# Half of an outer product from VectorE to ScalarE, and another order of the loads of the second layer's weights

## The reference

```python
X = np.fft.fft(x, axis=1); X = np.fft.fft(X, axis=2)      # x: (2, 3008, 256)
h = X.real.reshape(6016, 256) @ w_in                      # first layer, w_in: (256, 2048)
g = np.maximum(h, 0.0) ** 2
z = g @ w_out                                             # w_out: (2048, 256)
h = z @ w_in2                                             # second layer, same shapes
P = a[0] + a[1] * h + a[2] * h**2 + a[3] * h**3
Q = 1.0 + abs(b[0]) * abs(h) + abs(b[1]) * h**2
out = (P / (Q + 1e-06)) @ w_out2
```

## Time and profile before

| | |
|---|---|
| median of 3 runs | 1040.42 us (1040.05 to 1041.73) |
| profiled execution, its own time | 1043.1 us |
| its span | 1041.3 us |
| TensorE (PE) busy | 1003.2 us, 96% |
| VectorE (DVE) busy | 941.8 us, 90% |
| ScalarE (ACT) busy | 882.0 us, 85% |
| GpSimd (POOL) busy | 572.1 us, 55% |

### The profile page before, as it was taken

How to read it: one execution, slowest core, us unless ns; L and a number is a source line. 1 busy time by engine, 2 the same in 40 slices (tenths; PEclk the granted TensorE clock), 3 DMA queues, 4 the chain that set the end, 5 groups by cost and what they waited for, 6 DMA issues and landing times.

```text
span 1041.3 us, 13708 instructions
## 1 busy us (share of the span) xinstructions
PE 1003.2 (96%) x5098; PEld 848.1 (81%) x5098; DVE 941.8 (90%) x1040; ACT 882.0 (85%) x929; POOL 572.1 (55%) x305
## 2 busy tenths in 40 slices
PE   9999889999999999999999999999999999999875
PEld 8798778888888888888888888888888888788775
DVE  2368899999999999999999999999999999999997
ACT  2348879999899999899899999999999999898873
POOL 0143955656556556556556566566565565565342
PEclk9999989999999999999999999999999999999997
DMA  9766000001001001001001001001001000000000
GB/s 247 289 194 236 7 1 27 1 1 47 1 1 46 1 1 46 1 1 46 2 1 46 1 1 46 1 1 46 1 1 40 1 1 21 1 21 1 1 21 15
DMA packets 24174, 38.02 MB, mean 37 GB/s; under 512 B 1694, under 2 KB 18986, under 8 KB 23466
## 3 DMA queue, kind: packets, MB, share of 16 engines
q1 hardware_dynamic: 24060, 37.14, 11.3%
q10 hardware_dynamic: 48, 0.02, 0.0%
HBM read 25.31 MB, written 11.84 MB: 36 GB/s over the span
## 4 chain that ended last, share of the span: by engine, by line
DVE 45%; ACT 28%; issue 15%; PE 9%; POOL 2%; DMA 1%; DVEq 0%; ACTq 0%; SPq 0%
DVE den_s L725 9%; DVE den_s L738 9%; DVE den_s L736 9%; ACT seed_s L594 9%; ACT seed_s L591 8%; DVE g_value L742 8%; ACT minus_s L543 5%; DVE ps L690 4%; PE ps L805 3%; PE ps L825 2%; PE ps L814 1%; ACT g_value L575 1%; PE ps L868 1%; ACT g_value L549 1%; POOL w_in_lo L465 1%
## 5 line engine op out<-in xcount | busy, mean ns | idle before, releaser
L868 PE MATMUL ps<-g_hi,w_out_lo 128*128 128x512 f32 (+1 forms) x764 | 301.6, 395 | 17.3 <-POOL w_in_lo L500 8.0
L868 PE MATMUL ps<-g_hi,w_out_hi 128*128 128x512 f32 (+1 forms) x764 | 300.3, 393 | 0.0
L868 PE MATMUL ps<-g_lo,w_out_hi 128*128 128x512 f32 (+1 forms) x728 | 283.9, 390 | 0.0
L498 POOL CAST g_hi<-g_value 128x1024 fp32r<-128x1024 f32 x86 | 89.6, 1042 | 339.5 <-DVE g_value L742 339.5
L500 POOL TENSOR_TENSOR g_lo<-g_value,g_hi 128x1024 fp32r<-128x1024 f32 x86 | 207.3, 2411 | 6.9
L491 POOL TENSOR_TENSOR g_lo<-g_value,g_hi 128x1024 fp32r<-128x1024 f32 (+1 forms) x86 | 204.6, 2380 | 0.0
L868 PEld LDWEIGHTS ps<-g_hi,w_out_lo 128*128 128x128 f32 x764 | 145.9, 191 | 47.3 <-POOL w_in_lo L500 9.3
L868 PEld LDWEIGHTS ps<-g_hi,w_out_hi 128*128 128x128 f32 x764 | 145.2, 190 | 29.2
L868 PEld LDWEIGHTS ps<-g_lo,w_out_hi 128*128 128x128 f32 x728 | 137.9, 189 | 25.6
L581 ACT ACTIVATE den_s<-den_s 128x1024 f32<-128x1024 f32 x88 | 93.5, 1062 | 62.9 <-DVE den_s L725 62.8
L736 DVE SCALAR_TENSOR_TENSOR den_s<-den_s,seed_s 128x1024 f32<-128x1024 f32 x87 | 107.7, 1238 | 25.3 <-ACT seed_s L594 25.3
(11 more groups left out here) (118 smaller groups left out, 1894.2 us busy)
## 6 DMA issues: line engine op xcount, KB each, us to landing
x_s<-x SPq DMA_DIRECT2D x16, 384.0 KB, 7.2
out_t<-out_s SPq DMA_DIRECT2D x11, 512.0 KB, 5.7
w_out_unsplit_lo<-w_out SPq DMA_DIRECT2D x2, 2048.0 KB, 18.4
tw_s<-twiddle SPq DMA_DIRECT2D x1, 3012.0 KB, 17.3
y_hi_dram<-y_stage_hi SPq DMA_DIRECT2D x10, 256.0 KB, 3.7
y_lo_dram<-y_stage_lo SPq DMA_DIRECT2D x10, 256.0 KB, 4.5
w_in_raw<-w_in SPq DMA_DIRECT2D x1, 2048.0 KB, 10.5
w_in_unsplit_lo<-w_in SPq DMA_DIRECT2D x1, 2048.0 KB, 9.9
```

What stands on the lines that cost most here:

```text
L868: last = nc.tensor.matmul(acc[:, mb, 0:n], w[a][:, f, mb * P:(mb + 1) * P], g[c][:, i, 0:n], start=(f == 0 and j == 0), stop=(f == FB - 1 ...
```

## The change

Two things are changed. From unit 12 (SHARED) on, the second half (i = 1) of the outer product is written by ScalarE, as a copy with a per-partition scale, in step s for unit s + 1, right behind `square_relu(s)`. VectorE writes the first half, after a wait for ScalarE's. And SP issues w_in2 ahead of y of the second tile, in four transfers of 512 columns with a semaphore each; then comes w_out2, then that y. GpSimd waits for the quarter that it is about to split.

```diff
+SHARED = SKEW + 2
...
 # SP
+            for c in range(DFF // W_COLS):
+                cols = slice(c * W_COLS, (c + 1) * W_COLS)
+                sp.dma_start(w_in2_raw[:, :, cols], w_in2[:, cols].rearrange("(k p) f -> p k f", p=P)).then_inc(w_in2_loaded[c], 16)
+            load_w(w_out2_raw, w_out2, w_out2_loaded)
             load_y(1)
-            load_w(w_in2_raw, w_in2, w_in2_loaded)
-            load_w(w_out2_raw, w_out2, w_out2_loaded)
...
 # GpSimd
-            pool.wait_ge(w_in2_loaded, 16)
             for c in range(DFF // W_COLS):
+                pool.wait_ge(w_in2_loaded[c], 16)
...
 # ScalarE
+            act.wait_ge(w_col_ready, 1)
...
+            def outer_product(m):
+                t, n = m // UNITS, pairs(m // UNITS)
+                f = 2 * (m % UNITS) + 1
+                if m % UNITS == 0:
+                    act.wait_ge(u_loaded[t % Y_BUFS], 16 * (t // Y_BUFS + 1))
+                act.wait_ge(diff_done, m)
+                nc.scalar.activation(h1_plus(m)[:, 1, :], u_s[:, t % Y_BUFS, 0:n], ACT.Copy, scale=w_col[:, f:f + 1]
+                                     ).then_inc(act_outer_ready, 1)
...
                 square_relu(s)
+                if SHARED <= s + 1 < STEPS:
+                    outer_product(s + 1)
...
 # VectorE, in outer_product(m)
-                for i in range(2):
+                if m >= SHARED:
+                    dve.wait_ge(act_outer_ready, m + 1 - SHARED)
+                for i in range(2 if m < SHARED else 1):
...
 # TensorE
-                pe.wait_ge(outer_ready, 2 * m + 2)
+                pe.wait_ge(outer_ready, 2 * m + 2 if m < SHARED else SHARED + m + 1)
```

More of the change, by code:

```diff
@@ L216, in fft_moe_kernel @@
         y_stored = [sem(f"y_stored{n}") for n in range(STAGE_BUFS)]
-        w_in1_loaded, w_out1_loaded, w_in2_loaded, w_out2_loaded = (
-            sem(f"w_{n}_loaded") for n in ("in1", "out1", "in2", "out2"))
+        w_in1_loaded, w_out1_loaded, w_out2_loaded = (sem(f"w_{n}_loaded") for n in ("in1", "out1", "out2"))
+        w_in2_loaded = [sem(f"w_in2_loaded{c}") for c in range(DFF // W_COLS)]
         w_step, w_out1_ready, w2_ready = sem("w_step"), sem("w_out1_ready"), sem("w2_ready")
@@ L227, in fft_moe_kernel @@
         u_loaded = [sem(f"u_loaded{n}") for n in range(Y_BUFS)]
-        outer_ready = sem("outer_ready")
+        outer_ready, act_outer_ready = sem("outer_ready"), sem("act_outer_ready")
         plus_ready, minus_ready, minus_kept = sem("plus_ready"), sem("minus_ready"), sem("minus_kept")
```

## The result

| kernel | median of 18 runs | range | ratio to before, 95% interval |
|---|---|---|---|
| before | 1041.45 us | 1040.05 to 1044.77 | |
| after | 1045.11 us | 1043.05 to 1046.22 | 1.0028 [1.0019, 1.0036] |

The change costs 0.28%, some 2.9 us. The forecast was +1.6 us on 1040.42, and its range, 1036.5 to 1046.0, holds the time. The profiled execution of after spans 1043.1 us, that of before 1041.3. The changed lines stand 10 to 20 lower in the file: L725 is now L742, L567 and L575 are L580 and L588, L690 is L707, L747 is L764. ScalarE's new operation is L555.

What follows compares the result with a forecast made beforehand. The order of one step binds: VectorE's chain at 9.70 us, with 0.32 us slack in ScalarE's. +4.9 (stretch) + 0.3 (last steps) - 3.6 (loads) = +1.6 on 1040.42: 1042.0 us, range 1036.5 to 1046.0.

Steps and rivals of the forecast that it cites:

- Which chain sets the step: Normal step: VectorE's chain falls to 9.31 us, ScalarE's rises from 9.38 to 9.75 and sets it, against 9.70 before.
- Rival 4: VectorE's chain was the only bound and ScalarE hides the operation: about 1028 us, chance 0.04.
- The third bound: TensorE, 99.3% busy, could follow a shorter step only to about 9.63 us.
- The price d: Net delay of ScalarE's chain by the new operation between L551 and L567: 0.37 us, break-even 0.35.
- Rival 2: The new ScalarE operation is dear, d of 0.40 or more: 1044.4 us at 0.40, 1052 at 0.50; chance 0.13.
- The tile end and the copy step: The step ending a tile falls from 10.82 to 10.65 us; the step with L613, once a tile, takes 10.08.
- The last tile: Seven narrower steps behind the stretch, each given a normal step's price of 0.05 us: +0.3 us.
- The loads: Head: GpSimd's earlier splits shorten the steps of units 0 and 1 by 2.7 and 0.9 us: -3.6 us.
- rival 3: The loads bring nothing, by VectorE and GpSimd slowing each other or by unit 12's order: 1045.6 us, chance 0.07.
- Splits near 121: GpSimd's splits of w_in2 and w_out2 end near 121 us, against 127.25 before.
- the third read: Sign: the third L725 comes 3 to 5 us earlier than 145.09, or the prediction is wrong.
- its cover: y of the second tile lands near 99 us, TensorE first reads it at 102.90: 4 us to spare.

Runs made afterwards that it cites:

- extra_op: before plus one more ScalarE operation of the same shape at the change's place, into unused SBUF, VectorE keeping both halves: 1054.36 us, 1.0113.
- two_extra: before plus two such ScalarE operations at the change's place, into unused SBUF, VectorE as before: 1081.58 us in a single run.
- loads_only: after with only the loads' new order and quarters, VectorE writing both halves of the outer product: 1038.42 us, 0.9961 of before.
- z_lo_and_last: after, but ScalarE writes the second half only ahead of z's low part and, in the last tile, in every unit: 1035.44 us, 0.9931.
- early_12: loads_only with VectorE's halves of unit 12 made ahead of the first divide instead of behind it: 1039.22 us, 0.9971.
- tile_ends: after, but ScalarE's half only in one unit in eight, one step before the tile end, behind L588: 1037.77 us, 0.9962.
- one_transfer: loads_only with w_in2 still ahead of y but in one transfer with one wait: 1039.24 us in a single run.

## Why the prediction was right, and where its terms were off

- **Which chain sets the step: right.** L742 waits for L588 in each normal step with a handover of 0.10 to 0.12 us, and the 0.39 us freed on VectorE are not gained. extra_op gives the same 9.79 us with VectorE untouched. Rival 4, VectorE as the only bound (about 1028), is refuted by this and by two_extra. The third bound, TensorE at 9.63 us from its busy share, is not supported: extra_op has TensorE busy 99.33 of 100 us from 300 to 400 us, before 99.32, though its normal step is 0.10 us longer. So the share doesn't tell how much shorter a step TensorE could follow.
- **The price d: the step that was mis-sized.** "I take the middle, d = 0.37" took about half of 0.035 us off for PSUM as destination. The operation delays the next by 0.40 us, at the edge of the 0.32 to 0.40 outside which the prediction called itself wrong. The record does shorten (459 against 493 ns), but not the distance between starts. The estimate by the Trainium skill ("ScalarE: Activation LUTs", What ACT_TABLE_LOAD costs), 0.40, was met, and my 0.39 without the discount was too. The sentence of the Trainium skill that PSUM is the faster destination ("ScalarE: Activation LUTs", Step-by-step) agrees with the record's 34 ns; the queue behind gained nothing. With 0.40, 56 x 9.78 + 9 x 10.68 + 9 x 10.11 = 734.8, +7.1 against +7.3 measured (+4.9 forecast). Rival 2, the dear operation, is what happened there, though not for its reason, a wait and handover of the operation's own: two_extra's second operation costs 0.39 us, its distance to the next and nothing more.
- **The tile end and the copy step: right.** 10.70 against 10.65 forecast, 10.06 against 10.08.
- **The last tile: wrong in sign.** I gave its seven steps +0.05 each; from unit 76 to 85 the time fell by 1.55 us. Narrower ScalarE operations and a wait for TensorE stood there before, so ScalarE had room for the half, and VectorE's shorter chain counted. extra_op, which leaves VectorE its work, wins nothing (86.27). ScalarE's and VectorE's timelines, before and then after:

```profile
930.95 1.27 DVE L725 SCALAR_TENSOR_TENSOR den_s<-den_s,b_abs,ps 128x1024 f32<-128x1024 f32 x1
...
937.79 1.12 ACT L567 ACTIVATE den_s<-ps,coef_s 128x1024 f32<-128x1024 f32 x1 [0.22 <-PE ps L859]
...
940.41 1.27 DVE L725 SCALAR_TENSOR_TENSOR den_s<-den_s,b_abs,ps 128x1024 f32<-128x1024 f32 x1
```

```profile
931.78 0.41 ACT L555 ACTIVATE ps<-u_s,w_col 128x196 f32<-128x196 f32 x1
932.13 1.09 ACT L580 ACTIVATE den_s<-ps,coef_s 128x1024 f32<-128x1024 f32 x1
...
934.44 1.28 DVE L742 SCALAR_TENSOR_TENSOR den_s<-den_s,b_abs,ps 128x1024 f32<-128x1024 f32 x1
...
943.63 1.28 DVE L742 SCALAR_TENSOR_TENSOR den_s<-den_s,b_abs,ps 128x1024 f32<-128x1024 f32 x1
```

  A step is 9.46 us before and 9.19 after. The new operation delays the next by 0.35 us here (931.78 to 932.13). From L551 to L567 it was 1.08 us with the wait for TensorE, and from L564 to L580 it is 1.11 us without one, so that wait has absorbed nearly all of the operation.
- **The loads: right in kind, -3.6 forecast, -3.0 measured.** The first two steps brought 3.94 us (2.68 + 1.26) where I had 3.6; rival 3 is out. What I had in rival 3 alone, and at nothing in the sum, is that GpSimd's splits now reach further into the steps ahead of unit 0, where VectorE's L774 takes 2.30 us instead of 1.22 and a step of TensorE 4.48 instead of 4.22. From step 3 to unit 0 it is 40.63 us instead of 39.67: +1.0. "Splits near 121": 122.09. By one of its own signs the prediction was wrong, if by little: the third read was to come 3 to 5 us earlier than 145.09, and it came at 142.30, 2.8 us earlier. The clock still fell (0.77 from 130 to 135, against 0.50), and the stall at unit 12 was 4.14 us, "near 4" as forecast. y cost nothing; its cover is 103.68 - 99.0 = 4.7 us, 0.8 of it because TensorE now comes later, and that though SP stood 6.3 us in one issue on the way.
- **The sum.** +7.3 - 1.55 - 3.0 = +2.7 us by these segments, +2.9 by the ratio. Two errors of mine, d (2.4 too low) and the last tile (1.85 too high), nearly cancel, and the loads (0.6 too hopeful) add to the first. So that the sum came as near as it did is in part luck. The time was 1045.11 against 1042.0 forecast; some 1 us of that difference is the median of before itself, 1041.45 here.

**Open.** The last segment takes 80.2 to 82.5 us, in no order that follows the edits. The granted clock is below 1.00 in the last segment at differing times, but it doesn't order the executions: from 1010 to 1020 and from 1020 to 1030 us it is 0.75 and 0.74 in loads_only (80.3 us), and 1.00 and 0.83 in after (81.1 us). Over whole runs the mean granted clock goes with the time. Of 44 runs of before with a listed clock, the 20 at 0.990 to 0.993 took 1040.0 to 1041.8 us but for one (1043.0), and the 24 at 0.988 took 1042.1 to 1044.8 but for two (1040.5, 1041.9). Which of the two brings the other, and what starts it, was not tried. So z_lo_and_last's 1.2 us in the last tile can neither be claimed nor denied in the medians.

## What to carry to other kernels

Where three engines are all over 90% busy, measure the slack of the next chain before moving work: here it was 0.32 us and the operation moved cost 0.40. The place within the step decided the price: over 74 steps and with the same loads, 7.3 us ahead of what the other engine waits for, nothing behind it. The best use was the one step in eight where the engine relieved alone sets the length; relieved one step early, the gain was given back.

## What the runs showed of the hardware

- A 128x256 ScalarE copy with a per-partition scale has a record of 459 ns into PSUM and 493 into SBUF, and delays the next operation by 0.40 us in both cases.
- VectorE and GpSimd hold each other up. In after, L774 (two SBUF inputs) started at 93.95, GpSimd's subtraction ended at 95.16, and L774 took 1.08 us more than alone. GpSimd's next cast then took 2.03 us instead of 1.04. This agrees with the Trainium skill ("SBUF — State Buffer", SBUF: two separate sides): whichever of two such operations starts first holds a shared port pair for its whole length, and the other is blocked. What VectorE lost was the overlap with GpSimd's operation less 0.13 to 0.15 us: 1.21 us of overlap cost 1.08 (L774), 2.16 cost 2.02 (L738 of before at 128.41), 0.86 cost 0.72 (L749 of early_12), 0.33 cost 0.18 (L762 of tile_ends), and 0.10 cost nothing (L736 of before at 582.32).
- SP stood 6.27 us in the issue of y behind the w_in2 and w_out2 transfers; the same issue took 0.36 us ahead of them. With w_in2 in one transfer (one_transfer) it took 7.96 us, so the four transfers aren't what makes it long.
